# Spreading the fades by a product and an exponential, with part of the first expert weights moved to the input queue

## What is computed

```python
m_new = np.maximum(f_gate[:, :, t] + m, i_gate[:, :, t])
f_stab = np.exp(f_gate[:, :, t] + m - m_new)
i_stab = np.exp(i_gate[:, :, t] - m_new)
C = f_stab * C + i_stab * outer(v_t, k_t);  n = f_stab * n + i_stab * k_t
y[:, :, t] = sigmoid(o_gate) * (C @ q_t) / max(|n . q_t|, 1)
```

## Time and profile before

| | us |
|---|---|
| median of three runs | 407.49 |
| the profiled execution, its own time | 407.79 |
| its span, first to last instruction | 406.1 |
| last `attend` (step 23) begins | 162.3 |
| `expert_first` begins | 176.3 |
| first output tile of the feed-forward layer | 212.6 |

### The profile page before, as it was taken

The page is one execution under the profiler, slowest core; times in us unless marked ns, Lnnn a source line. Parts: engine busy times, 40 slices in busy tenths (PEclk is TensorE's granted clock), DMA queues, the critical chain, the costliest instruction groups (busy, mean ns, idle before and its releaser), DMA issues.

```text
span 406.1 us, 9533 instructions
## 1 busy us (share of the span) xinstructions
PE 374.9 (92%) x3484; PEld 315.6 (78%) x3484; DVE 238.7 (59%) x556; ACT 220.7 (54%) x436; POOL 78.6 (19%) x119
## 2 busy tenths in 40 slices
PE   2989978898799879999999999999999999999996
PEld 2667756576667657634569999999999999999996
DVE  8745756745856576441158756556556556556553
ACT  3554546455546565312048866666666666666662
POOL 4255645354544544000000000000000000000000
PEclk9996999998989999999999999999999999999999
DMA  6389999999999998996900001001001001001001
GB/s 179 90 245 254 268 283 254 243 263 265 260 260 241 254 257 283 350 363 217 364 6 2 0 2 65 2 2 65 0 0 65 0 0 65 0 0 65 0 2 65
DMA packets 31816, 56.83 MB, mean 140 GB/s; under 512 B 3524, under 2 KB 20548, under 8 KB 31524
## 3 DMA queue, kind: packets, MB, share of 16 engines
q1 hardware_dynamic: 28308, 45.84, 40.5%
q10 hardware_dynamic: 3472, 10.51, 9.6%
HBM read 51.83 MB, written 4.42 MB: 139 GB/s over the span
## 4 chain that ended last, share of the span: by engine, by line
PE 68%; DMA 13%; SPq 11%; DVE 4%; issue 2%; ACT 1%; ACTq 0%; DVEq 0%
DMA row_x<-cum_scratch 12%; PE heads_banks L1109 7%; PE high_banks L1111 7%; PE high_banks L1110 7%; PE high_banks L1109 7%; PE heads_banks L1110 7%; PE heads_banks L1111 7%; PE low_banks L1097 5%; SPq L393 3%; PE low_banks L1032 2%; PE heads_banks L823 2%; PE low_banks L802 2%; PE low_banks L1013 2%; PE low_banks L959 2%; SPq L351 2%
## 5 line engine op out<-in xcount | busy, mean ns | idle before, releaser
L747 ACT ACTIVATE relu_h<-low_banks 128x512 f32<-128x512 f32 x96 | 57.4, 598 | 60.5 <-PE low_banks L1097 60.1
L1422 DVE CAST sq_hi<-sq_h 128x512 fp32r<-128x512 f32 x96 | 41.0, 427 | 66.7 <-ACT sq_h L752 66.1
L1424 DVE TENSOR_TENSOR sq_lo<-sq_h,sq_hi 128x512 fp32r<-128x512 f32 x96 | 66.5, 692 | 3.3
L752 ACT ACTIVATE sq_h<-relu_h 128x512 f32<-128x512 f32 x96 | 60.6, 632 | 3.1
L1111 PE MATMUL high_banks<-wo_hi,sq_lo 128*128 128x320 f32 x192 | 59.3, 309 | 0.0
L1109 PE MATMUL high_banks<-wo_hi,sq_hi 128*128 128x320 f32 x192 | 59.3, 309 | 0.0
L1110 PE MATMUL high_banks<-wo_lo,sq_hi 128*128 128x320 f32 x192 | 59.3, 309 | 0.0
L1109 PE MATMUL heads_banks<-wo_hi,sq_hi 128*128 128x320 f32 x192 | 59.3, 309 | 0.0
L1110 PE MATMUL heads_banks<-wo_lo,sq_hi 128*128 128x320 f32 x192 | 59.1, 308 | 0.0
L1111 PE MATMUL heads_banks<-wo_hi,sq_lo 128*128 128x320 f32 x192 | 59.1, 308 | 0.0
L1152 DVE TENSOR_TENSOR att_w<-low_banks,att_w 128x512 f32<-128x512 f32 x48 | 30.9, 685 | 37.2 <-POOL att_w L538 21.0
(11 more groups left out here) (177 smaller groups left out, 548.8 us busy)
## 6 DMA issues: line engine op xcount, KB each, us to landing
w_sb<-in_w SPq DMA_DIRECT2D x8, 1280.0 KB, 12.5
w_a<-in_w ACTq DMA_DIRECT2D x16, 512.0 KB, 9.6
kv_in<-in_kv SPq DMA_DIRECT2D x24, 320.0 KB, 13.8
qk_in<-in_qk SPq DMA_DIRECT2D x24, 256.0 KB, 7.2
fade_b<-fade_scratch SPq DMA_DIRECT2D x40, 128.0 KB, 8.3
o_in<-in_o_gate SPq DMA_DIRECT2D x24, 160.0 KB, 13.6
out<-out_sb SPq DMA_DIRECT2D x5, 640.0 KB, 3.2
wo_raw<-in_w_out SPq DMA_DIRECT2D x4, 640.0 KB, 12.0
```

Of the source, the lines that this page charges most:

```text
L747: act.activation(relu_h[:, slot], bank[slot][:, :], ACT.Relu).then_inc(relu_done, 1)
L752: act.activation(sq_h[:, slot], relu_h[:, slot], ACT.Square).then_inc(sq_done, 1)
L1422: dve.tensor_copy(sq_hi[:, slot], sq_h[:, slot]).then_inc(hi_done, 1)
L1424: dve.tensor_tensor(sq_lo[:, slot], sq_h[:, slot], sq_hi[:, slot].bitcast(F32), ALU.subtract).then_inc(lo_done, 1)
```

## The change

The fade no longer passes through DRAM. `store_fades`, `load_fades`, their scratch tensor and their semaphores go, and so does the exponential over the [32, 768] tile. Instead TensorE multiplies `row_x` of the step with a constant 0/1 tile `cum_pick` (`spread_fade`, 42 rows, 128 columns of weights, 512 streamed columns, in bank 1), which puts the high and low parts' sum on all 128 partitions; ScalarE takes its exponential into `fade_b` (`raise_fade`). Bank 1 is shared with `decay`'s second matmul and `logit`, which now wait for that exponential. GpSimd scales q after the mask instead of before it, and makes `cum_pick` at the start.

ScalarE's queue now issues only w1's rows 0 to 255 of experts 0 to 5, one 512 KB piece in each odd step (12 DMAs). Rows 0 to 255 of experts 6 and 7 (two DMAs of 1 MB) and the last 64 rows of all experts (one DMA of 2 MB) are issued by SyncE behind the last step's inputs, ahead of w2.

```diff
             def load_rows(b, c):
                 at_least(sp, decay_logs, 2 * (n - ROW_RING + 1))
+                at_least(sp, fade_logs, rescales(*before(b, c, ROW_RING)))
...
-            sp.wait_ge(gate_act, A_FADE)
-            store_fades(0)
...
-            sp.wait_ge(rows_stored, 16)
-            load_fades(0, 1)
-            for b in range(1, B):
-                store_fades(b)
...
-            sp.wait_ge(rows_stored, 16 * (B + 2))
-            load_fades(0, 2)
-            load_fades(0, 3)
+            sp.wait_ge(rows_stored, 32)
...
-                    if far[1] > 0 and far != (0, 3):
-                        load_fades(*far)
                     load_qk(sp, *far)
...
-                if n == STEPS - 3:
-                    load_w2(0)
-
+            for e in range(W1_EARLY, E):
+                sp.dma_start(w1_a[:, e], w1[e, 0:2 * P, :].rearrange("(k p) n -> p k n", p=P)).then_inc(w1_loaded, 16)
+            sp.dma_start(w1_b[:, :, :], w1[:, 2 * P:DM, :].rearrange("e r (h n) -> (r h) e n", h=2)).then_inc(w1_loaded, 16)
+            load_w2(0)
...
             def scale_q(b, c):
-                pool.wait_ge(fades_loaded[fade_slot(b, c)], 32 * ((rescales(b, c) - 1) // FADE_RING + 1))
+                pool.wait_ge(fade_ready, rescales(b, c))
...
+                mask(b, c)
                 if c > 0:
                     scale_q(b, c)
-                mask(b, c)
...
+            def raise_fade(b, c):
+
+                act.wait_ge(fade_logs, rescales(b, c))
+                at_least(act, q_scaled, rescales(b, c) - FADE_RING)
+                pb, pc = (b, c - FADE_RING) if c > FADE_RING else (b - 1, c - FADE_RING + NC - 1)
+                at_least(act, carry_half, (NC - 2) * pb + min(pc, NC - 2))
+                act.activation(fade_b[:, fade_slot(b, c)], fade_ps, ACT.Exp).then_inc(fade_ready, 1)
...
-                if n % 5 > 0 and n - n // 5 <= len(W1_PARTS):
-                    e, k = W1_PARTS[n - n // 5 - 1]
+                if n % 2 == 1 and n // 2 < 2 * W1_EARLY:
+                    e, k = n // 4, n // 2 % 2
                     act.dma_start(w1_a[:, e, k], w1[e, P * k:P * (k + 1), :]).then_inc(w1_loaded, 16)
...
                     copy_heads(b, c)
+                    if c < NC - 1:
+                        raise_fade(b, c + 1)
...
+                    if r == 1:
+                        at_least(pe, fade_ready, rescales(*before(b, c)))
...
+            def spread_fade(b, c):
+
+                pe.wait_ge(decay_exp, 2 * step(b, c) + 2)
+                if (b, c) == (0, 1):
+                    pe.wait_ge(pick_placed, 1)
+                rows = slice(0, QUAD + H + 2)
+                pe.matmul(bank[1][:, :], cum_pick[:, :, :].rearrange("p r d -> p (r d)"), row_x[rows, :, step(b, c) % ROW_RING],
+                          start=True, stop=True).then_inc(fade_logs, 1)
...
             def logit(b, c):
+                if b < B - 1 or c < NC - 1:
+                    pe.wait_ge(fade_ready, rescales(*after(*after(b, c))))
...
                     route(rb, c, 1 - half)
+                if cur and c < NC - 1:
+                    spread_fade(b, c + 1)
                 if nxt:
                     score(*after(b, c))
```

More of the change, by code:

```diff
@@ L106, in build_program @@
         row_half = sb("row_half", [P, KC + 1])
+        cum_pick = sb("cum_pick", [QUAD + H + 2, 2, DP], F32R)
         with ExitStack() as own:
@@ L120, in build_program @@
             keyw = sb("keyw", [NS, S], stack=own)
-            fade = sb("fade", [NS, S], stack=own)
             cum_parts = sb("cum_parts", [NS, 2, S], F32R, stack=own)
@@ L220, in build_program @@
         src_loaded = [sem(f"src_loaded{i}") for i in range(2)]
-        fades_loaded = [sem(f"fades_loaded{i}") for i in range(FADE_RING)]
         qk_loaded = [sem(f"qk_loaded{i}") for i in range(3)]
@@ L315, in build_program @@
         G_START, G_M, G_FM, G_LOGF, G_CUM, G_SRC, G_CUMLO, G_SRCLO, G_KEYW = range(1, 10)
-        A_CUM, A_FADE, A_SRC, A_KEYW = range(1, 5)
+        A_CUM, A_SRC, A_KEYW = range(1, 4)
         decay_bank, score_bank = bank[0:2], bank[2:4]
@@ L329, in build_program @@
         head_rows_in = att_w[0:QUAD + H, 1, 0:HP]
-        W1_PARTS = [(e, k) for e in range(E) for k in range(2)]
+        W1_EARLY = 6
+        W1_DMAS = 2 * W1_EARLY + E - W1_EARLY + 1
         def half_of(r, j):
@@ L384, in load_rows @@
                     sp.dma_start(row_x[p0:p0 + 2, :, s].bitcast(F32), rows).then_inc(rows_loaded[s], 16)
-            def load_fades(b, c):
-                s = fade_slot(b, c)
-                at_least(sp, q_scaled, rescales(b, c) - FADE_RING)
-                pb, pc = (b, c - FADE_RING) if c > FADE_RING else (b - 1, c - FADE_RING + NC - 1)
-                at_least(sp, carry_half, (NC - 2) * pb + min(pc, NC - 2))
-                for r in range(2):
-                    row = fade_dram[b, c:c + 1, HP * L * r:HP * L * (r + 1)]
-                    sp.dma_start(fade_b[DP * r:DP * (r + 1), s].rearrange("p h t -> p (h t)"), row.broadcast_to([DP, HP * L]))\
-                        .then_inc(fades_loaded[s], 16)
-            def store_fades(b):
-                to = fade_dram[b].rearrange("c (h t) -> h c t", h=H)
-                sp.dma_start(to, fade[H * b:H * (b + 1), :].rearrange("h (c t) -> h c t", t=L)).then_inc(rows_stored, 16)
             def load_src(b):
@@ L547, in _ @@
             pool.memset(carry[:, :, :, :], 0.0).then_inc(cleared, 1)
+            pool.memset(cum_pick[:, :, :].bitcast(F32), 1.0).then_inc(pick_made, 1)
+            for side in range(2):
+                pool.wait_ge(pick_made, side + 1)
+                pool.affine_select(out=cum_pick[:, :, :], in_=cum_pick[:, :, :].bitcast(F32), compare_op=ALU.is_ge, fill=0.0,
+                                   base=(-H, H + 1)[side], pattern=[[(-QUAD, QUAD)[side], 2], [0, DP]],
+                                   channel_multiplier=(1, -1)[side]).then_inc((pick_made, pick_placed)[side], 1)
             mask(0, 0)
@@ L617, in load_w1 @@
                     act.wait_ge(rows_direct, 96)
-                    act.wait_ge(rows_stored, 16 * (B + 2))
+                    act.wait_ge(rows_stored, 32)
                     act.wait_ge(keyw_turned, 1)
-                if n % 5 > 0 and n - n // 5 <= len(W1_PARTS):
-                    e, k = W1_PARTS[n - n // 5 - 1]
+                if n % 2 == 1 and n // 2 < 2 * W1_EARLY:
+                    e, k = n // 4, n // 2 % 2
                     act.dma_start(w1_a[:, e, k], w1[e, P * k:P * (k + 1), :]).then_inc(w1_loaded, 16)
-                if n > 0 and n % 5 == 0:
-                    for e in range(2 * (n // 5 - 1), 2 * (n // 5)):
-                        rest = w1[e, 2 * P:DM, :].rearrange("r (h n) -> (r h) n", h=2)
-                        act.dma_start(w1_b[:, e], rest).then_inc(w1_loaded, 16)
             def dispatch_exp(rb):
@@ L663, in _ @@
             act.activation(cum_parts[:, 0], cum[:, :], ACT.Copy).then_inc(gate_act, 1)
-            act.activation(fade[:, :], cum[:, :], ACT.Exp).then_inc(gate_act, 1)
             act.wait_ge(gate_vec, G_SRC)
```

10 lines of the change are left out of this document (7 added, 3 removed).

## The result

| | before | after |
|---|---|---|
| median, us | 408.95 (407.35 to 410.79) | 392.06 (391.72 to 393.35) |
| ratio of after to before | | 0.959, 95% interval 0.953 to 0.965 |
| the profiled execution, its own time | 407.79 | 391.97 |
| its span | 406.1 | 390.3 |
| last `attend` begins (L816, L821) | 161.7 | 145.6 |

The change makes the kernel 16.9 us faster by the medians. The forecast was 9.7, a median of 397.8, and its range ended at 393.5. The span became 15.8 us shorter (406.1 to 390.3), and the same 15.8 is there at the first output tile: all of the gain is made before the feed-forward layer, and none is lost in it. The other 1.1 us comes from the fourth run of before, 410.79, which moved its median from 407.49 to 408.95; the forecast of 9.7 is best held against 15.8.

The account below looks back on a forecast made before the run. Full DMA engines were taken to bound the attention, losing 20.9 us. Less 8.6 for spreads, 0.8 first-chunk waits, 1.0 small waits and 0.8 late weights, the gain was 9.7: median 397.8, range 393.5 to 403.5 (0.81).

Parts of the forecast that it names:

- The loss to transfers, 20.9 us: Attention: 20 steps took 129.4 us against 108.5 without transfer waits; all 20.9 us were taken to go.
- The clean steps of 108.5 us: Attention: the 20 steps from 27.75 to 157.16, summed by kind of step without waits for transfers.
- after, 186 GB/s, 70% of it: Attention after the change: 1.09 MB in a step of about 5.85 us, 70% of the full DMA rate.
- The spread, 8.6 us: TensorE in the attention: 20 added matmuls of 512 columns at 0.43 us each, priced like `decay`.
- The other bound: Lower price for a spread, from the feed-forward layer's 512-column matmul: 0.22 us each, 4.4 us in all.
- The first chunk's waits, 0.8 us: TensorE in a batch's first chunk waits 0.2 to 0.3 us for the exponentials, four times at most.
- The allowance of 1.0 us for small waits: Attention: 1.0 us set aside for small waits on ScalarE, GpSimd and others that the new exponentials might cause.
- The slack of 0.76 us: Plain attention step: chain from `attend` through exponential and scaling takes 2.8 us, TensorE's work between 3.56.
- rivals B and C: Attention: spread's chain of exponential and scaling binds. B: gain 3, 405, 5%; C: slower than before, about 412, 3%.
- The tail, 0.8 us: Behind the attention: w1 and w2 queue behind the last inputs and arrive late, taking back 0.8 us.
- rival E: Cheaper than forecast: spread at 0.22 us and no late weights, gain 14.7, 392.8 us; chance 8%.
- Rival D: Attention: waits come from in-order queue latency, not load, so half remain; gain 1 to 2, 406; chance 4%.

Follow-up runs that it names:

- distinct_128: Kernel before, its fades read from w_in (wrong numbers) by one DMA of 128 rows to all partitions per step; 395.36 us, ratio 0.970.
- w1_late_only: Kernel before with only w1's issues moved as in the change, fades still loaded through DRAM; 397.07 us, ratio 0.973.
- spread_x4: Changed kernel with each spread's matmul done four times into the same bank; 405.87 us, 13.8 us above the changed kernel.
- product_only: Changed kernel with w1 left where it was before, on ScalarE's queue in every step; 392.06 us, ratio 0.961.
- w1_all_late: Changed kernel with all of w1 (10 MB) issued behind the last inputs, none during the attention; 407.07 us, ratio 1.000.

## Why the prediction was wrong

**The loss to transfers, 20.9 us: right in size, wrong in its cause.** The clean steps of 108.5 us came out within 0.6: the measured 112.4 less 17 spreads at 0.23 and three waits of 0.2 is 107.9, so 21.5 us were lost. But the argument was 1576 KB a step against 260 GB/s, taken as the rate of mixed inputs. That rate was that of the fades' form: 283 to 289 with the same bytes to all partitions. 128 KB to 64 neighbouring partitions costs more than its bytes. Of the 20.9 us some 13 go with the form alone (one DMA to all partitions in place of two to the halves): in distinct_128 the same 20 steps take 116.4 us (27.75 to 144.18) instead of 129.4.

```profile
27.75 0.50 PE L790 MATMUL low_banks<-row_x,row_y 10*128 10x512 f32 x2
...
46.64 0.59 PE L790 MATMUL low_banks<-row_x,row_y 10*128 10x512 f32 x2 [0.23 <-ACT xT L603]
...
144.18 0.49 PE L790 MATMUL low_banks<-row_x,row_y 10*128 10x512 f32 x2
```

It leaves 7.9 us of the loss. The steps from 27.75 to 46.64 take 18.9 us, against 14.94 clean, so about half of the 7.9, 4.0, is lost in these first steps.

The forecast was right to take the whole 20.9 for gone, since the change removes these loads altogether. Its step "after, 186 GB/s, 70% of it" was near (203 and 0.67 measured). Who had reasoned from it that fewer bytes are what matters would have built w1_late_only, and got two thirds of it.

**The spread, 8.6 us: the step that failed, by 4.0 us.** 0.43 us is the distance from `decay` to `attend`, and `decay` is two matmuls; the text says so itself ("both matmuls together") and then gave the price of the pair to one matmul. The other bound, from the feed-forward layer's 512 columns, was right: the text has 0.22 (5% of 406.1 over 96 is 0.21), and spread_x4 gives 0.23. 20 times 0.23 is 4.6. The reason given for the higher bound, that operands change on both sides, had no row behind it.

**The first chunk's waits, 0.8 us:** 0.21 at 84.48; 0.6 in all, three times.

**The allowance of 1.0 us for small waits:** the last fade step waits 0.29 (145.63), no other. 0.7 too much. The slack of 0.76 us that the text gave the chain is near what after's timeline has. In one second chunk the scaling of q ends at 92.06 + 1.28 = 93.34 and `attend` begins at 94.10, 0.76 later; over all fade steps it is 0.42 to 1.94 us, but for the last with 0.10.

```profile
92.06 1.28 POOL L514 TENSOR_TENSOR q_fade<-qk_in,fade_b 128x512 f32<-128x512 f32 x1 [1.10 <-ACT fade_b L585]
...
94.10 0.67 PE L821 MATMUL heads_banks<-q_fade,carry 64*64 64x128 f32 x16
```

So rivals B and C did not come. The order on GpSimd was judged rightly, but in one sentence and without a price; undone, it costs 11.9 us.

**The tail, 0.8 us:** 0.24. The first w2 was issued at 134.96 (forecast 137.5; the attention was shorter). The late w1 had landed by 143.3 (its last DMA, issued at 134.45, takes 8.8 us), where the forecast had about 158 for it; the rates of that stretch, 380 and 399 GB/s, stand against the 310 assumed:

```profile
135.00:140.00 5.00, 4.81 (x66) 3.06 (x61) 3.98 (x10) 2.41 (x6) 2.21 (x3) 1.00 0.96 380
140.00:145.00 5.00, 5.00 (x76) 4.03 (x77) 1.65 (x6) 3.42 (x9) 1.98 (x3) 1.00 1.04 399
```

Only the pair of halves is stretched, 4.75 for 4.51 us. SyncE's queue of after, the issues of w1, w2 and w_in (answering to the earlier trace rows):

```profile
132.42 1.99 SPq L454 DMA_DIRECT2D w_a<-in_w  x2
134.45 0.47 SPq L455 DMA_DIRECT2D w_b<-in_w  x1
134.96 33.44 SPq L399 DMA_DIRECT2D w_sb<-in_w  x8
...
171.40 0.52 SPq L472 DMA_DIRECT2D win_sb<-in_w_in  x1
```

TensorE's timeline, the second product of the experts:

```profile
176.76 4.75 PE L1041 MATMUL low_banks<-w_sb,hidT 128*32 128x320 f32 x64 [0.25 <-ACT hidT L714]
```

The row of w2 alone, 359 GB/s, was nearer than 310. By the Trainium skill's figure of about 358 ("DMA: Bandwidth & Descriptors", "Where 436 GB/s comes from") the tail was free, which came closer than the 0.8. But the figure bounds neither side here: the 380 and 399 of w1 lie above it, and the attention's own loads ran far below it at full share, between 245 and 289 GB/s by their form. Product_only, whose w1 is in earlier, has 4.51 there, but its last `attend` begins 0.24 us later (145.87), and its time is the same: moving w1 was worth nothing, for or against. The forecast never asked what each half of the change would bring alone.

**Sum by the measured terms:** 20.9 - 4.6 - 0.6 - 0.3 - 0.24 = 15.2, or 15.8 with the 21.5 in place of 20.9, and the span moved by 15.8. This is rival E, which stood at 8% with 392.8. The range was said to hold most of E, yet it ended at 393.5, above E's own figure. The terms of the forecast erred the same way, each taken at the careful end; the spread alone is 4.0 of the 6.1 us by which the span missed. Rival D (latency of the queue, not load) fell: k and v land in 3.7 us instead of 13.8. Of what the last part named as signs, the share (0.67), the full clock, the missing waits and the last `attend` spoke for the mechanism (its second part at 146.2, where the 152 of the forecast, 162.3 less 10.5, was reckoned from that part). One was not met: 0.4 us between the starts of L796 and L807; the timeline has 74.30 and 74.31. The first plain steps with a spread take 4.9 us (28.09 to 32.98) instead of the 5.2 that was forecast; one without a spread takes 4.75 as before (43.63 to 48.38).

## What to carry to other kernels

Price an added instruction by a row of one such instruction; where the row holds a pair, halve it, and where two bounds lie a factor of two apart, look at which of them counts the same thing. A DMA rate read from full engines belongs to the forms of the transfers in it: before concluding that bytes bind, look which partitions each load reaches, above all for loads of half of them. Where an engine gets a new wait, look first at what is queued behind it: the order of two lines on GpSimd decided about 12 us here.

## What was not expected of the hardware

- 256 KB a step to 64 neighbouring partitions at a time cost 16 to 22 us over product_only, to all 128 partitions 2, to even and odd ones 5, at full DMA share in each case: 245 to 263 against 283 to 285 GB/s from 40 to 140 us.
- One DMA whose source's outermost dimension is 2 took the kernel from 408 to 472 us, with the DMA engines' mean share down to 0.59.
- Behind the attention's inputs, with w1 and w2, the engines moved 363 to 399 GB/s, and 405 in w1_all_late from 140 to 160 us, against at most 289 at full share from 40 to 140 us.
- The stall of 3.52 us in w1_all_late was paid for twice: behind it the granted clock was 0.60 over six us, and 32 matmuls took 6.03 us instead of 3.64.
- A float32r matmul of 512 streamed columns on 42 rows takes 0.23 us of TensorE when others follow, though its own row says 0.50.
- Open: why 64 partitions in two DMAs of even and odd ones are still 3.3 us slower than one of 128 (here the number of DMAs and their order changed together), and whether the late start of step 3's inputs is what makes the 4.0 us of the first steps in distinct_128, and what the other 3.9 of its 7.9 are; none of these was tried apart. No view shows whether it is ports that make the difference between the partitions.
